# A planned schedule for the short slots: high parts and weight splits ahead of a chunk's steps on ScalarE, VectorE's gate behind the phases, other slot lengths

## The reference

```python
mag = sqrt(a_re**2 + a_im**2);  scale = minimum(mag, 0.999) / (mag + 1e-6)
for t in range(768):                       # per batch and head
    S = (a * scale)[t] * S + outer(k[t], v[t])     # S complex, 48 x 48
    y[t] = q[t] @ real(S)
x = y.transpose(0, 2, 1, 3).reshape(3072, 384)
h = x @ w1_in;  x = (h * clip(h + 3, 0, 6) / 6) @ w1_out
h = x @ w2_in;  out = (maximum(h, 0) + alpha * minimum(h, 0)) @ w2_out
```

## Time and profile before

| what | before |
| --- | --- |
| median of three runs | 1003.53 us (1002.75 to 1005.13) |
| the profiled execution | 1003.23 us, its span 1001.5 us |
| TensorE busy | 964.9 us (96%) |
| VectorE, ScalarE, GpSimd busy | 584.1, 502.0, 268.2 us |
| mean granted TensorE clock | 0.998 |
| means by line, 103 to 349 us | state's two operations 0.54 and 0.68 us, key copy 0.48, `leave` 0.79, split on ScalarE 0.62 |

### The profile page before, as it was taken

The page is one execution under the profiler, slowest core; times in us unless marked ns, Lnnn a source line. Parts: engine busy times, 40 slices in busy tenths (PEclk is TensorE's granted clock), DMA queues, the critical chain, the costliest instruction groups (busy, mean ns, idle before and its releaser), DMA issues.

```text
span 1001.5 us, 17747 instructions
## 1 busy us (share of the span) xinstructions
PE 964.9 (96%) x6858; PEld 868.4 (87%) x6858; DVE 584.1 (58%) x1049; ACT 502.0 (50%) x907; POOL 268.2 (27%) x251
## 2 busy tenths in 40 slices
PE   2899989999999999999999999999999999999998
PEld 2788978999999999999999998888888888888786
DVE  6868886777777767777662345444434444344332
ACT  7767886777777777776643543322222122222111
POOL 0000222222232322322222333332333333323332
PEclk9999999999999999999999999999999999999999
DMA  7853334333444333444320801023060060230000
GB/s 218 216 151 95 96 86 109 94 98 80 111 101 126 95 97 80 108 108 111 88 49 1 308 1 56 0 74 85 1 151 8 0 158 1 68 91 1 32 0 32
DMA packets 86661, 84.72 MB, mean 85 GB/s; under 512 B 31152, under 2 KB 81328, under 8 KB 86192
## 3 DMA queue, kind: packets, MB, share of 16 engines
q1 hardware_dynamic: 86576, 83.58, 31.3%
HBM read 55.10 MB, written 14.19 MB: 69 GB/s over the span
## 4 chain that ended last, share of the span: by engine, by line
PE 82%; ACT 5%; DVE 4%; SPq 3%; DMA 2%; issue 2%; ACTq 0%; DVEq 0%
PE op L1263 12%; PE hp L1264 12%; PE op L1264 11%; PE hp L1263 11%; PE op L1265 11%; PE hp L1265 11%; PE yp L1251 3%; PE gp L1258 2%; PE gp L1230 2%; PE yp L1230 2%; PE hp L1286 2%; PE op L1311 2%; DMA a_sb<-a_in 1%; DMA st<-rows 1%; ACT L608 1%
## 5 line engine op out<-in xcount | busy, mean ns | idle before, releaser
L584 POOL TENSOR_TENSOR g_lo<-gated,g_hi 128x512 fp32r<-128x512 f32 (+2 forms) x240 | 266.0, 1108 | 726.2 <-ACT g_hi L679 726.2
L679 ACT ACTIVATE g_hi<-gated 128x512 fp32r<-128x512 f32 (+2 forms) x240 | 126.3, 526 | 314.7 <-DVE gated L969 273.7
L965 DVE TENSOR_SCALAR gate<-hp,alpha_sb 128x512 f32<-128x512 f32 x96 | 72.0, 750 | 209.5 <-PE hp L1265 209.5
L954 DVE SCALAR_TENSOR_TENSOR gated<-gate,hp 128x256 f32<-128x256 f32 (+1 forms) x160 | 75.2, 470 | 134.1 <-ACT gate L672 133.5
L1263 PE MATMUL op<-g_hi,wb_hi 128*128 128x256 f32 (+1 forms) x432 | 137.5, 318 | 2.3 <-ACT out_sb L684 1.2
L1263 PE MATMUL hp<-x_hi,wa_hi 128*128 128x256 f32 (+1 forms) x432 | 134.8, 312 | 0.3 <-DVE x_lo L918 0.2
L1265 PE MATMUL op<-g_hi,wb_lo 128*128 128x256 f32 (+1 forms) x432 | 132.4, 306 | 0.0
L1264 PE MATMUL hp<-x_lo,wa_hi 128*128 128x256 f32 (+1 forms) x432 | 132.3, 306 | 0.0
L1265 PE MATMUL hp<-x_hi,wa_lo 128*128 128x256 f32 (+1 forms) x432 | 132.3, 306 | 0.0
L1264 PE MATMUL op<-g_lo,wb_hi 128*128 128x256 f32 (+1 forms) x432 | 132.3, 306 | 0.0
L672 ACT ACTIVATE gate<-hp,half 128x256 f32<-128x256 f32 (+1 forms) x160 | 81.2, 507 | 98.7 <-PE hp L1265 89.2
(11 more groups left out here) (115 smaller groups left out, 1652.7 us busy)
## 6 DMA issues: line engine op xcount, KB each, us to landing
st<-prod SPq DMA_DIRECT2D x96, 145.1 KB, 3.0
raw<-a_in SPq DMA_DIRECT2D x4, 2304.0 KB, 15.2
a_sb<-a_in SPq DMA_DIRECT2D x24, 288.0 KB, 3.7
qk_sb<-qk_in SPq DMA_DIRECT2D x24, 288.0 KB, 3.7
rows<-prod SPq DMA_DIRECT2D x48, 96.8 KB, 2.4
st<-rows SPq DMA_DIRECT2D x48, 96.8 KB, 2.8
v_pad<-v_in SPq DMA_DIRECT2D x24, 192.0 KB, 3.5
x_raw<-x SPq DMA_DIRECT2D x6, 768.0 KB, 16.2
```

What stands on the lines that cost most here:

```text
L584: pool.tensor_tensor(g_lo[:, at, 0:wide], gated[:, at * UT:at * UT + wide], g_hi[:, at, 0:wide].bitcast(F32), ALU.subtract).then_inc(glo_d ...
L679: act.activation(g_hi[:, at, 0:wide], gated[:, at * UT:at * UT + wide], ACT.Copy).then_inc(ghi_done, 1)
L954: dve.scalar_tensor_tensor(out=gated[:, to], in0=gate[:, at], scalar=1.0, in1=hp[:, n % 2, 0:wide], op0=ALU.min, op1=ALU.mult).then_inc(ga ...
L965: dve.tensor_scalar(gate[:, at], hp[:, n % 2, 0:wide], 0.0, alpha_sb[:, m:m + 1], ALU.min, ALU.mult).then_inc(gate_done, 1)
```

## The change

Five things change, all in the short slots (and ahead of them for the splits). (1) ScalarE runs `high`, the item's splits and `leave` directly behind the gate piece and the key copy, ahead of waves, logs, squares, inverses, x high and angle; the table load for the logs comes ahead of them, `copy_ends` right behind. (2) VectorE's gate stands between phases and fractions; (3) the masks of item "cf" come ahead of the backward scan. (4) Slot lengths go from 6, then eight times 7, then 8, 7, 7, 8 to 6, 8, 8, 8, then eight times 7, then 6; the eight-item plan gets "k" and "b" in items of their own. (5) The 24 splits go to items 2 to 19, two in every third item, in an order worked out from the item from which a block is free. Nothing is computed otherwise, and the long slots keep their order.

```diff
-         8: ("a", "cf", "deos", "glv", "hi", "j", "kb", "")}
+         8: ("a", "cf", "deos", "glv", "hi", "j", "k", "b")}
-LENGTHS = (6,) + 8 * (7,) + (8, 7, 7, 8) + 2 * (5, 5, 6) + (5, 6, 6)
+LENGTHS = (6, 8, 8, 8) + 8 * (7,) + (6,) + 2 * (5, 5, 6) + (5, 6, 6)
-W_ITEM = 3
+def usable(block):
+    return -(-(block[1] + 1) * WPC // DM) if block[0] else block[2] * WPC // P + 1
+def split_plan():
+    left = [b for q in range(NQ) for b in A_BLOCKS[q]] + B_BLOCKS
+    plan = {}
+    for n in range(2, 2 * MT_FF):
+        plan[n] = [b for b in left if usable(b) <= n][:1 + n % 3 // 2]
+        left = [b for b in left if b not in plan[n]]
+    assert not left
+    return plan
...
 def splits_at(n):
-    return range(max(0, n - W_ITEM), min(max(0, n + 1 - W_ITEM), len(W_ORDER)))
+    return [W_ORDER.index(b) for b in SPLIT_PLAN.get(n, [])]
...
         (ScalarE)
+            def behind_gate(n):
+                if n + GSTEP >= MT_FF:
+                    high(n + GSTEP)
+                for w in splits_at(n):
+                    split_w(w)
+                if n % MT_FF == MT_FF - 1:
+                    leave(n // MT_FF)
             for n in range(ALONE):
                 gate_of(n + GSTEP)
+                for w in splits_at(n):
+                    split_w(w)
...
             for steps, n, c0, c1, c2, c3 in places():
                 gate_of(n + GSTEP)
+                if "a" in steps and keeps:
+                    copy_k(c0, 0)
+                if "c" in steps and keeps:
+                    copy_k(c0, 1)
+                if is_short(c0):
+                    if "c" in steps and c2 is not None:
+                        act.preload_act_table_set("natural_log_exp_and_others")
+                    behind_gate(n)
+                    if "c" in steps and c1 is not None:
+                        copy_ends(c1)
+                if "a" in steps and c1 is not None:
+                    waves(c1)
+                if "c" in steps and c2 is not None:
+                    logs(c2, is_short(c0))
...
-                if n + GSTEP >= MT_FF:
-                    high(n + GSTEP)
-                if "c" in steps and c1 is not None:
-                    copy_ends(c1)
-                for w in splits_at(n):
-                    split_w(w)
-                if n % MT_FF == MT_FF - 1:
-                    leave(n // MT_FF)
+                if not is_short(c0):
+                    (the same, without splits)
         (VectorE)
                 if "a" in steps and c1 is not None:
                     phases(c1)
-                    fractions(c1)
+                    if not is_short(c0):
+                        fractions(c1)
                 gate1(n + GSTEP)
+                if is_short(c0):
+                    if "a" in steps and c1 is not None:
+                        fractions(c1)
+                    if "f" in steps:
+                        mask(c0, 0)
+                        mask(c0, 1)
                 if "c" in steps and c1 is not None:
                     backward(c1)
...
-                if "f" in steps:
+                if "f" in steps and not is_short(c0):
```

More of the change, by code:

```diff
@@ L77 @@
 B_BLOCKS = [(1, n) for n in range(NWI)]
-W_ORDER = [b for q in range(NQ) for b in A_BLOCKS[q] + B_BLOCKS[(0, 1, 3, 6)[q]:(1, 3, 6, NWI)[q]]]
-W_ITEM = 3
+def usable(block):
[8 more added lines that the diff above has]
+    return plan
+SPLIT_PLAN = split_plan()
+W_ORDER = [b for n in SPLIT_PLAN for b in SPLIT_PLAN[n]]
 NRP = 12
@@ L604, in squares, with logs @@
                 act.activation(t_sq[:, :, :, :], a_sb[:, c % 2, :, :, :], ACT.Square).then_inc(squares_set, 1)
-            def logs(c):
-                if c > 0:
+            def logs(c, loaded=False):
+                if c > 0 and not loaded:
                     act.preload_act_table_set("natural_log_exp_and_others")
```

## The result

The changed kernel takes **1021.32 us** (median of four runs, 1020.81 to 1023.51) against 1004.25 us for the kernel before in the same session: 1.0176 times as long, 95% interval 1.0155 to 1.0196. It is slower by some 17 us, as forecast (1019 us, range 1004 to 1027). Its profiled execution took 1021.29 us, span 1019.6 us, mean clock 0.993. TensorE has 652.7 us to go from the end of the short slots in both kernels (1019.6 - 366.91 and 1001.5 - 348.84), so in the profiled executions all of the loss, 18.1 us there, lies ahead of that point, as the prediction had it.

What follows compares the result with a forecast made beforehand. TensorE bounds the kernel, the ScalarE-VectorE lap close behind; the longer lap was to take over: +12.8 us in slots 6 to 14 and +2.9 in slots 3 to 5, +15.7 on 1003.2, gives 1019 us, range 1004 to 1027.

Steps and rivals of the forecast that it cites:

- the lap: ScalarE and VectorE from one chunk's phases to the next: 21.13 to 23.0 us in seven-item slots, bounds 22.6 and 23.4.
- X high's price: Item "h": x high starts later behind the waiting high part, delaying VectorE's x low, state and next gate: +0.9 us.
- the gain of item "a": At the phases, the low part on GpSimd no longer runs over their scans: an estimate of -0.4 us, or 0.
- the inverses: Item "glv": they queue behind the high part, which waits for VectorE's gate, so ScalarE's next gate comes later: +1.8 us.
- The low part off the phases: GpSimd's low part moves ahead of the phases' scans: -0.4 us, or 0 if it falls on the fractions.
- Slots 6 to 14: The seven- and six-item slots, bound by the lap: 203.9 us against 191.1 for the same work before, +12.8.
- slot 12: A batch's first chunk, which saves one state operation, about 0.6: a lap of 22.4 us.
- Slot 14: The slot now of six items, which saves one of VectorE's gates, 0.3: 22.7 us.
- Slots 3 to 5: Eight-item slots with denser splits: 27.6, 26.6 and 27 us, ending +2.9 us later, bounds -8 and +6.
- slot 5: Last chunk: unit 2's first matmul waits for x low, 19.4 us into the slot against 13.5 without a wait; 27 us.
- the rival with the clock: Longer TensorE waits in every slot lower the clock; shows only where it lasts: 1030 us and more, chance 0.04.
- Slot 3: Unit 1's first matmul waits for x low about 1.3 later, its first output some 0.5 for emptied sums: 27.6 us.
- The faster rival: TensorE stays the bound, early stalls go, laps stay under 21.1: 998 us (993 to 1001), chance 0.11.

Runs made afterwards that it cites:

- Experiments 1 to 3: Three runs: experiment 1, experiment 2, and the changed kernel with high part, splits and `leave` behind the step only for inverses, x high and angle, 1001.13 us.
- experiments 5 to 7: The changed kernel with the high part behind one step only, inverses, x high or angle in turn: 1014.0, 1014.42 and 1014.94 us.
- experiment 2: The kernel before with ScalarE's changed order alone; lengths, split dates and VectorE's order as before: 1022.48 us, ratio 1.02.
- experiment 9: The changed kernel, its order kept, with slot lengths 6, 7, 8, six of 7, 8, three of 7: 1014.93 us, ratio 1.0114.
- Experiment 11: The kernel of experiment 8 with one split an item in items 3 to 26, as before: 1001.87 us, ratio 0.9987.
- experiment 1: The changed kernel with ScalarE's order of before, steps ahead of the high part; all else stays changed: 1005.72 us, ratio 1.0016.
- experiment 8: The changed kernel, high part behind inverses, x high and angle, slot lengths 6, 7, 8, six of 7, 8, three of 7: 999.41 us.
- experiment 12: The kernel of experiment 8 with an item moved from slot 4 to slot 5: 996.46 us, ratio 0.9933.

## Why the prediction was right

**Which bound takes over.** The forecast was that ScalarE's high parts, ahead of the steps, lengthen the lap over TensorE's 21.13 us. Experiments 1 to 3 show it: the loss goes with ScalarE's order and comes with it alone, and putting back three of its positions takes away all of it. The laps of slots 7 to 10 were 22.65, 22.79, 22.63 and 22.72 us against a forecast of 23.0 with bounds of 22.6 and 23.4: the right mechanism, 0.3 us too large. X high's price (0.66 for 0.9), the gain of item "a" (0.54 for 0.4) and the inverses (1.7 for 1.8) were the terms that were off. That prices on the lap can be summed and turned into time holds only so far: one price taken away alone is partly eaten up by TensorE or by waits for rows (experiments 5 to 7), and masks and slot lengths changed the time beside the laps (experiments 2 and 9).

**The low part off the phases.** The phases' scans took 1.24 us for three instead of 1.66, and the forward scans, which now have a low part beside them (252.98 to 253.90), 1.54 instead of 1.05. The loss is covered: those scans run beside the angle's table load, to the end of which nothing waits for them. The Trainium skill (SBUF — State Buffer, "SBUF: two separate sides") has the shared port pair held by one of the two for a whole instruction, and by it the fractions, which start first, keep their time. The trace agrees: the fractions start 0.23 us ahead of the low part (234.54 and 234.77) and take 0.56 us, as before. The lap of 22.7 us is near the lower end of 22.6 too, but x high's smaller price has the larger part in that.

**Slots 6 to 14.** Forecast 203.9, measured 204.5 us, but not by the same terms. The nine laps add up to 202.3 us (0.3 less in each full slot). That of slot 12 was 23.29 instead of 22.4, for two reasons. The emptying of the sums stands ahead of x high there (314.55 and 315.24 us), so that x low comes 1.98 us after VectorE's gate instead of 1.29. And at the slot's start, behind TensorE's wait of 2.3 us for rows, ScalarE waits 0.9 and 0.4 us for TensorE. Slot 14 was 24.9 instead of 22.7 us. I had not costed the wait for x low before unit 6 there: x high stands in the very item of that unit's first hidden product, and TensorE waited 3.2 us, up to 361 us. The clock of 0.93 in that slot is another 1.7 us. So that the sum came within 0.6 us is luck in part: the laps were too large, the last slot too small.

**Slots 3 to 5.** Forecast 27.6, 26.6 and 27, measured 27.56, 27.14 and 29.06. In slot 5 x low came as said, 152.56 - 133.32 = 19.2 us into the slot (forecast 19.4); the wait was 4.2 us and not 19.4 - 13.5 = 5.9, since TensorE itself got there 1.5 us later. What was mis-sized is what follows: 9.8 us to the slot's end, forecast 7.6. TensorE in the changed kernel, at that place:

```profile
152.56 0.58 PE L1304 MATMUL hp<-x_hi,wa_hi 128*128 128x256 f32 x1 [4.20 <-DVE x_lo L950]
152.94 0.41 PE L1305 MATMUL hp<-x_lo,wa_hi 128*128 128x256 f32 x1
...
157.42 0.34 PE L1305 MATMUL hp<-x_lo,wa_hi 128*128 128x256 f32 x1
157.60 0.27 PE L1306 MATMUL hp<-x_hi,wa_lo 128*128 128x256 f32 x1
157.71 0.28 PE L1304 MATMUL hp<-x_hi,wa_hi 128*128 128x256 f32 x1
```

From 152.56 to 157.42 us the matmuls stand 0.21 us apart, behind that 0.12: 4.9 us at 1.2 GHz instead of 2.4 (the granted clock is 0.51 from 152.6 to 157.6 us), and 23 matmuls take 2.1 us longer than at 0.12. That is the missing 2 us. I had counted the clock in slot 6 of the kernel before (1.7 us), and called it hidden under a lap of 23.0. In slot 5 it isn't: the lap itself waits for TensorE there, ScalarE's gate pieces 5.0 us in two places between 150 and 175 us. So a small part of the rival with the clock came true beside the forecast: a lower clock behind a wait isn't always hidden.

**The splits.** Slot 3 came out to 0.04 us, and that is luck: TensorE's two waits there were 0.98 and 0.27 us, where some 1.5 and 0.5 were forecast, and it was busy for 26.31 us instead of 25.85. Experiment 11 suggests only that dense splits are worth something on the better order.

**The faster rival** said that early stalls would go and laps stay under 21.1. Its first half is real and smaller than the 7 us: slots 3 to 5 gained 3.2 us in experiment 1, and slots 6 to 14 lost 5.4. The second half fell with laps of 22.7 us.

**What stays open.** The parts don't add up in a plain way. ScalarE's order alone costs 2.0%, all but that order 0.2%, and both together 1.8%. Masks ahead of the scan probably save time under the new order (experiment 2), and the changed lengths cost some 6 us under it against those of experiment 9; no run has the masks alone, or the lengths of the kernel before, beside the rest of the change, and the sum wasn't taken apart further.

## What to carry to other kernels

Where two engines in program order hand a tile back and forth, work queued between the two halves of the exchange is free cover; putting the second half first makes each engine stand still for the other's latency, and such waits add up along the lap. Work out the lap of the two engines, not their busy share (VectorE was busy 58% of the span), and compare it with the bounding engine's time for the same stretch. Such prices give the size of a lap; what the time gains is less when another engine or a transfer is close behind. And look for the place where a result that takes long falls into the very item of its use: other slot lengths alone were worth 6 us in the changed kernel, and one item moved between two slots 3 us in the last one.

## What the runs showed of the hardware

A wait of TensorE can cost more than itself. Behind waits of 4.2 us (the changed kernel) and 2.9 us (experiment 8) the granted clock was at the lower level, with matmuls 0.21 us apart instead of 0.12; the first case lasted 4.9 us and cost 2.1. In experiment 12, with no wait over 1.4 us for rows, the profiled execution kept the clock at 1.00 on average. The length of a wait alone doesn't tell: behind 1.6 us at 275.8 us in the changed kernel the clock was 0.66 for the next 5 us, behind 2.4 us at 153.6 us in experiment 11 it was 1.00.

An operation of 3 columns on VectorE (the floor of the ends) took 0.53 us beside a GpSimd operation, instead of 0.17: it ended at 249.73 us, the GpSimd operation at 249.70. In that run, with the angle first, it took 0.52 us in the median of ten; in the changed kernel, 0.17 in the median of nine. So a very short instruction can pay for a neighbour too.
